# Attention rebuilt around transposed q and k: two heads per step on the two halves of the PE rows

## The chip, the cores and the metric

One core of one Trainium2 chip runs the whole program. The metric is device time in microseconds (us), the median of several executions. TensorE is PE in the profile (its weight loads are PEld), VectorE is DVE, ScalarE is ACT, GpSimd is POOL, and SyncE, which issues most of the DMAs, is SP.

## The reference

Three stages run after each other on B = 2 batches of S = 768 tokens. Only the first changes. It is attention with H = 8 heads of D = 64, n_global = 8 and n_local = 96:

```python
scores = scale * np.matmul(q, k.transpose(0, 1, 3, 2))
is_global = pos[None, :] < int(n_global)
is_local = (rel >= 0) & (rel < int(n_local))
keep = is_global | is_local
dist = np.where(is_global & ~is_local, float(n_local), np.abs(rel))
scores = np.where(keep, scores - slopes * dist, -1000000000.0)
a = np.exp(scores - np.max(scores, axis=-1, keepdims=True))
a = a / (np.sum(a, axis=-1, keepdims=True) + 1e-09)
return np.matmul(a, v)
```

The result x (1536 rows of 512) then goes through a mixer (x + x U V along the sequence, a layer of 512 to 2048 to 512) and through a layer of 8 experts of which each token takes one.

## The kernel before

**Attention** works on 8 pairs of heads. A pair has 6 blocks of 128 queries, and each block of each head is one step: STEPS = 12 steps a pair, 96 in all. A query block t > 0 looks at a window of 256 keys: the first 32 keys (which hold the global ones), the last 96 keys of block t - 1, and the 128 of block t. Block 0 has 128 keys. All engines run the same loops (`pairs`: two counted loops with two pairs in the body) and wait on semaphores whose values are computed in registers.

q and k arrive with tokens on the partitions. `load_qk` brings a pair in rows of 64 numbers, `turn_qk` transposes it on PE (L1156, 12 transposes a pair), and `keep_qk` copies it out of PSUM twice: ACT writes the fp32r rounding (L1244, L1247), and DVE writes the remainder (L1339, L1344). k is written once per window, so that each step finds its 256 keys side by side. q has a copy for each head in which the other head's 64 rows are zero, so that every score matmul contracts over 128 rows.

A step then runs so:

- `scores` on PE: three fp32r passes (high by high, high by low, low by high; `passes`, L452) of 128 x 256 into one of two PSUM banks.
- `score` on DVE (L1356): adds the bias of the head (from POOL, L1494) and takes the row minimum of the negated scores.
- `exponentials` on ACT (L1254), which also accumulates the row sums (the read of the accumulator is an instruction of its own).
- `turn_probs` on PE, TURN_LAG = 2 steps later: two fp32 transposes (L1173).
- `keep_turned`: a copy out of PSUM, on ACT for one head (L1261), on DVE for the other (L1364).
- `weigh` on PE, WEIGH_LAG = 4 steps later: two fp32 matmuls with 64 columns of v (L1189, L1190). The trace shows an fp32 matmul as two weight loads and two matmuls.
- twice a pair, `invert` and `normalise` (L1383) on DVE write the quotient to x.

Beside this POOL splits one unit of w_ch1 (128 x 1024) a pair into rounding (L1477) and remainder (L1479) and issues the DMA of the next unit itself.

**At the start** POOL builds index tiles, DVE turns n_global and n_local into numbers (L1306 to L1316; `path_ready`), then makes the distance tile in ten operations (L1319 to L1329; `dist_done`), and POOL multiplies it by each head's slope. With n_global up to 32 and n_local up to 97 the engines take the windowed path; it is the one that runs here.

**After attention** PE starts the mixer with 12 fp32 matmuls (L496), once `attn_done` is set. The mixer and the experts are not touched by the change, but for where the split units of w_ch1 come from.

Of the kernel before, what the change touches and what calls it, by code (L numbers as in the profile page):

```python
# [11 lines left out]
F32 = mybir.dt.float32  # L12
F32R = mybir.dt.float32r
# [30 lines left out]
def build(nc, q, k, v, n_global, n_local, moe_U, moe_V, w_ch1, w_ch2, w_gate, w_local, w1, w2, out):  # L44
    B, H, S, D = q.shape
# [4 lines left out]
    R = moe_U.shape[1]  # L50
# [13 lines left out]
    WIN = 2 * P  # L64
    HALF = TB // 2
    STEPS = 2 * TB
    CREDIT = STEPS + 1
    TURN_LAG = 2
    WEIGH_LAG = 4
    BATCHES = 4  # L70
# [6 lines left out]
    with ExitStack() as ctx:  # L77
# [17 lines left out]
        limits = sb("limits", [P, 2, 2], I32)  # L95
# [7 lines left out]
        qs = sb("qs", [P, TB, 2, D], F32, attn)  # L103
        ks = sb("ks", [P, TB, 2, D], F32, attn)
        vs = [sb(f"vs{i}", [P, TB, 2 * D], F32, attn) for i in range(2)]
        va = [sb(f"va{i}", [P, TB - 1, 2 * D], F32, attn) for i in range(2)]

        q_parts = sb("q_parts", [P, 2, 2, 2, S], F32R, attn)
        dist = sb("dist", [P, 3 * P], F32, attn)
        bias = [[sb(f"bias{i}{h}", [P, 3 * P], F32, attn) for h in range(2)] for i in range(2)]  # L110
        TS = [sb(f"TS{i}", [P, WIN], F32, attn) for i in range(3)]
        PR = [sb(f"PR{i}", [P, WIN], F32, attn) for i in range(3)]
        PT = [sb(f"PT{i}", [P, WIN], F32, attn) for i in range(4)]
        low = sb("low", [P, 2, STEPS], F32, attn)
        total = sb("total", [P, 2, STEPS], F32, attn)
        inv = sb("inv", [P, 2, STEPS], F32, attn)
        attn.close()
        (glob, near), (rel, key) = bias

        full = ExitStack()  # L120
        f_q = sb("f_q", [P, 2, D], F32, full)
        f_k = sb("f_k", [P, TB, 2, D], F32, full)
        f_v = sb("f_v", [P, TB, 2, D], F32, full)
# [20 lines left out]
        k_parts = sb("k_parts", [P, 2, 2, TB, WIN], F32R, turned_k)  # L144
# [63 lines left out]
        cleared = sem("cleared")  # L208
        setup = sem("setup")
        q_in = sem("q_in")  # L210
        k_in = sem("k_in")
        v_in = [sem(f"v_in{i}") for i in range(2)]
        bias_ready = sem("bias_ready")
        tr_done = sem("tr_done")
        tr_act = sem("tr_act")
        tr_dve = sem("tr_dve")
# [58 lines left out]
        raw_first = sem("raw_first")  # L275
# [5 lines left out]
        score_bank, turn_bank, out_bank, tr_bank = bank[0:2], bank[2:4], bank[4:6], bank[6:8]  # L281


        def width(s):
            return P if s < 2 else WIN

        def windows(dst, src, half, part):


            of = src.rearrange("p (t n) -> p t n", t=HALF)  # L290
            t0, t1 = HALF * half, min(HALF * (half + 1), TB - 1)
            if part == 0:
                yield dst[:, t0:t0 + HALF, P:WIN], of
                return
            yield dst[:, t0 + 1:t1 + 1, GLOB:P], of[:, 0:t1 - t0, P - SPAN:P]
            if half == 0:
                yield dst[:, 1:TB, 0:GLOB], of[:, 0:1, 0:GLOB].to_broadcast([P, TB - 1, GLOB])

        def pairs(eng, body):


            with eng.Fori(0, B) as b:
                with eng.Fori(0, H // 4) as g:
                    m = b * (H // 4) + g
                    for par in range(2):
                        body(b, g, m, par, 2 * m + par)

        LAST = B * H // 2 - 1
        PASSES = B * H // 4


# [14 lines left out]
        def full_sp(sp):  # L326
            def load(t, b, g, m):
                wait_loop(sp, f_free, m + 1)
                for h in range(2):
                    head = 2 * g + h  # L330
                    view = "a p t d -> p (a t) d"
                    for dst, src in ((f_k, k), (f_v, v)):
                        sp.dma_start(dst[:, :, h, :], src.rearrange("b h (t p) d -> (b h) p t d", p=P)[
                            bass.ds(b * H + head, 1), :, :, :].rearrange(view)).then_inc(f_in, 16)
                    sp.dma_start(f_q[:, h:h + 1, :], q.rearrange("b h (t p) d -> (b h t) p d", p=P)[
                        bass.ds((b * H + head) * TB + t, 1), :, :].rearrange("a p d -> p a d")).then_inc(f_in, 16)

            full_steps(sp, load)

        def full_pe(pe):  # L340
            def step(t, b, g, m):
                wait_loop(pe, f_in, 96 * (m + 1))
                pe.transpose(bank[0][:, 0:P], f_q[:, :, :].rearrange("p h d -> p (h d)"), ident[:, :])
                for i in range(TB):
                    last = pe.transpose(bank[1 + i // 4][:, (i % 4) * P:(i % 4 + 1) * P],
                                        f_k[:, i, :, :].rearrange("p h d -> p (h d)"), ident[:, :])
                last.then_inc(f_pe, 1)
                for h in range(2):
                    part = slice(h * D, (h + 1) * D)
                    if h == 0:  # L350
                        wait_loop(pe, f_dve, FULL_T * (t + 1) + FULL * m + 3)
                    else:
                        wait_loop(pe, f_dve, FULL_T * (t + 1) + FULL * m + 3 + FULL_H)
# [1178 lines left out]
```

## Time and profile before

| | |
|---|---|
| median of 3 runs | 689.23 us (688.92 to 689.52) |
| span of the profiled execution | 689.6 us |
| attention, from the first score matmul to x | 21.41 to 137.58 us |
| mixer from | 138.34 us |
| PE busy, weight loads busy | 90%, 79% of the span |

The span runs from the first to the last instruction of the profiled execution. Its rows are in microseconds from that start. The end of a matmul is modelled in such a profile; the starts are what to count with.

### The profile page before, as it was taken

Reading aid. Unit: us, or ns where it says so; the run is one execution under the profiler, and the core shown is the slowest. Engines: PE = TensorE matmul, PEld = TensorE weight load, DVE = VectorE, ACT = ScalarE, POOL = GpSimd, SP = SyncE. Lnnn points to the kernel's source line nnn. Section 1 sums busy time; section 2 is a strip of 40 time slices with the busy share of each in tenths; the row PEclk is TensorE's granted clock in tenths of the full one; section 3 lists DMA queues with packets and bytes.
Section 4 is the critical chain, followed back from the end, with each engine's and each line's share of the span. In section 5 each row is a group of like instructions: output and inputs, shape, how many; then the busy total and the mean of one; then the engine's idle time right before and its main releaser. Section 6 shows DMA issues by size and latency. Waiting matters only on the chain.

```text
span 689.6 us, 11540 instructions
## 1 busy us (share of the span) xinstructions
PE 621.2 (90%) x3430; PEld 541.6 (79%) x3431; DVE 308.2 (45%) x670; ACT 254.1 (37%) x554; POOL 96.6 (14%) x145
## 2 busy tenths in 40 slices
PE   0899899989999999999999999925899998999994
PEld 0789889938999998989998999824677876887883
DVE  5688888624332212220222011483665447574521
ACT  1677788613221111111111201321655346464411
POOL 6634433000000000000000000001112111212111
PEclk9999999999999999999999999955999999999998
DMA  8965676001111100010001000234684528654310
GB/s 209 201 151 118 135 150 142 1 0 62 61 62 62 47 0 1 1 46 1 1 1 46 1 1 1 72 126 151 209 284 155 185 70 284 242 200 159 115 43 21
DMA packets 72175, 65.78 MB, mean 95 GB/s; under 512 B 53807, under 2 KB 53807, under 8 KB 72144
## 3 DMA queue, kind: packets, MB, share of 16 engines
q1 hardware_dynamic: 64800, 50.87, 25.3%
q0 software_dynamic: 4320, 13.90, 6.3%
q10 hardware_dynamic: 3024, 0.61, 0.6%
q8 instruction: 18, 0.29, 0.2%
q14 instruction: 13, 0.11, 0.1%
HBM read 59.07 MB, written 7.08 MB: 96 GB/s over the span
## 4 chain that ended last, share of the span: by engine, by line
PE 82%; DVE 6%; issue 4%; DMA 3%; ACT 2%; SPq 1%; DVEq 0%; POOL 0%; ACTq 0%; POOLq 0%
PE bank L452 65%; PE bank L900 3%; PE bank L1173 2%; PE bank L1190 2%; PE bank L496 2%; PE bank L1156 2%; DMA raw<-in_moe_w_dram 2%; PE bank L1189 2%; ACT hs L955 1%; DVE q_parts L1339 1%; PE bank L515 1%; PE bank L524 1%; DVE wbuf L595 1%; PE bank L844 1%; DMA limits<-in_n_local_dram 1%
## 5 line engine op out<-in xcount | busy, mean ns | idle before, releaser
L452 PE MATMUL bank<-uT,wbuf 128*128 128x384 f32 x768 | 144.8, 336 | 1.5 <-DVE uT L670 1.5
L452 PE MATMUL bank<-wbuf,hid 128*128 128x512 f32 x576 | 145.1, 396 | 0.0
L452 PEld LDWEIGHTS bank<-uT,wbuf 128*128 128x128 f32 x768 | 136.2, 188 | 7.0 <-issue 1.7
L703 DVE SCALAR_TENSOR_TENSOR hid<-bank,hid 128x384 fp32r<-128x384 f32 x64 | 35.7, 557 | 214.9 <-ACT hid L644 214.9
L452 PEld LDWEIGHTS bank<-wbuf,hid 128*128 128x128 f32 x576 | 106.0, 188 | 20.6 <-issue 0.7
L644 ACT ACTIVATE hid<-bank 128x384 fp32r<-128x384 f32 x64 | 31.5, 492 | 230.0 <-PE bank L452 230.0
L595 DVE TENSOR_TENSOR wbuf<-raw,wbuf 128x1024 fp32r<-128x1024 f32 x72 | 85.1, 1221 | 27.3 <-ACT wbuf L591 26.5
L452 PE MATMUL bank<-wbuf,xT 128*128 128x512 f32 x360 | 93.1, 410 | 1.7 <-DVE xT L985 1.7
L591 ACT CAST wbuf<-raw 128x1024 fp32r<-128x1024 f32 x72 | 72.9, 1047 | 41.4 <-PE bank L452 20.4
L452 PE MATMUL bank<-wbuf,hT 128*128 128x512 f32 x360 | 86.0, 394 | 0.0
L452 PEld LDWEIGHTS bank<-wbuf,xT 128*128 128x128 f32 x360 | 69.6, 197 | 16.3 <-issue 2.1
L452 PEld LDWEIGHTS bank<-wbuf,hT 128*128 128x128 f32 x360 | 66.6, 189 | 13.5
L452 PE MATMUL bank<-k_parts,q_parts 128*128 128x256 f32 (+1 forms) x288 | 57.9, 312 | 2.0 <-DVE k_parts L1344 2.0
L1254 ACT ACTIVATE PR<-TS,low 128x256 f32<-128x256 f32 (+1 forms) x96 | 47.3, 492 | 25.9 <-DVE low L1356 24.1
L1356 DVE CUSTOM_DVE_ANT_0 TS<-bank,bias 128x256 f32<-128x256 f32 (+1 forms) x96 | 38.1, 397 | 19.3 <-PE bank L452 13.4
L1020 POOL IOTA rev<- 128x96 f32 x1 | 0.3, 288 | 323.6 <-PE bank L452 323.6
L452 PEld LDWEIGHTS bank<-k_parts,q_parts 128*128 128x128 f32 x288 | 41.6, 196 | 2.5 <-issue 2.4
L1173 PE MATMUL bank<-ident,PR 128*128 128x128 f32 x176 | 36.5, 281 | 0.2
L955 ACT ACTIVATE hs<-bank 128x512 f32<-128x512 f32 x30 | 17.9, 597 | 46.1 <-PE bank L452 44.5
L1055 POOL DMA_INDIRECT out_dram<-ys,give x15 | 16.1, 1075 | 108.3 <-DVE ys L1011 108.3
L1190 PE MATMUL bank<-vs,PT 128*128 128x64 f32 x160 | 30.9, 275 | 0.0
L997 DVE TENSOR_TENSOR hT<-bank,hT 128x512 fp32r<-128x512 f32 x30 | 20.7, 689 | 21.6 <-ACT hT L961 21.4
(177 smaller groups left out, 622.1 us busy)
## 6 DMA issues: line engine op xcount, KB each, us to landing
raw<-in_moe_w_dram SPq DMA_DIRECT2D x64, 512.0 KB, 4.1
raw<-in_moe_w_ch_dram POOLq DMA_DIRECT2D x12, 512.0 KB, 5.9
qs<-in_q_dram SPq DMA_DIRECT2D x16, 192.0 KB, 5.5
ks<-in_k_dram SPq DMA_DIRECT2D x16, 192.0 KB, 4.5
vs<-in_v_dram SPq DMA_DIRECT2D x16, 192.0 KB, 2.6
mixed<-x SPq DMA_DIRECT2D x12, 256.0 KB, 2.1
raw<-in_moe_w_ch_dram SPq DMA_DIRECT2D x4, 512.0 KB, 3.5
va<-in_v_dram SPq DMA_DIRECT2D x16, 120.0 KB, 4.1
```

The costliest lines, as they stand in the source:

```text
L452: last = pe.matmul(dst, lhs[a], rhs[b_], start=start and i == 0, stop=stop and i == 2)
L591: act.copy(w[:, 0, i, :], raw[:, i % RAW, :]).then_inc(hi_split, 1)
L595: dve.tensor_tensor(w[:, 1, i, :], raw[:, i % RAW, :], w[:, 0, i, :].bitcast(F32), ALU.subtract).then_inc(lo_split, 1)
L644: act.activation(hid[i % 2][:, 0, :], bank[3 + i % 2][:, 0:BN], ACT.Relu).then_inc(hid_hi, 1)
L703: dve.scalar_tensor_tensor(hid[i % 2][:, 1, :], bank[3 + i % 2][:, 0:BN], 0.0, hid[i % 2][:, 0, :].bitcast(F32), ALU.max, ALU.subtract).th ...
L900: last = pe.transpose(bank[5 + half][:, c * P:(c + 1) * P], hs[:, half, c * P:(c + 1) * P], ident[:, :])
L955: act.activation(hs[:, half, :], bank[3 + half][:, :], ACT.Relu).then_inc(e_relu, 1)
L997: dve.tensor_tensor(hT[:, 1, half * NE // 2:(half + 1) * NE // 2, :], bank[5 + half][:, :].rearrange("p (c t) -> p c t", c=NE // 2), hT[:, ...
L1173: last = pe.transpose(turn_bank[s % 2][:, c * P:(c + 1) * P], PR[s % 3][:, c * P:(c + 1) * P], ident[:, :])
L1190: last = pe.matmul(dst, PT[s % 4][:, P:WIN], vs[par][:, t, vcol], start=False, stop=True)
L1254: act.activation(PR[s % 3][:, 0:w], TS[s % 3][:, 0:w], ACT.Exp, bias=low[:, par, s:s + 1], scale=-1.0, accum_out=total[:, par, s:s + 1]).t ...
L1356: dve.tensor_tensor_reduce(TS[s % 3][:, 0:w], score_bank[s % 2][:, 0:w], bias[par][s % 2][:, col], -SCALE, 3.0e38, ALU.add, ALU.min, low[: ...
```

## The change

The host hands over other layouts: q and k of a pair transposed (128 rows: head 0 on partitions 0 to 63, head 1 on 64 to 127), v with a column of ones behind each head and with the shifted windows already laid out, both limits and both gates in one array each. On the chip:

- Both heads of a query block are one group: 6 groups a pair, 48 in all, written out without loops; waits are on constants.
- `turn_qk` and `keep_qk` are gone. POOL makes rounding and remainder of q and k from SBUF (`split_qk`); for the first 256 columns of the first pair ACT and DVE do it.
- A score matmul contracts over the 64 rows of its head. The keys are not copied into windows: for t > 0 each pass is a matmul of 32 keys and one of 224, for each head, so a group has 12 score matmuls (6 at t = 0) into two PSUM banks, of four.
- The row sums come from the ones column of v in the `weigh` matmuls (65 columns), so `exponentials` no longer accumulates, and the reciprocal is part of `normalise`.
- `keep_turned` copies both heads at once (512 columns), on ACT for four groups of six, on DVE for two.
- The roundings of w_ch1 are made by ACT (`first_hi`); POOL makes only the remainders, and SP issues their DMAs.
- The distance tile takes five DVE operations, of which four come behind the limits.

```diff
+            def load_qk(n):
+                sp.dma_start(k_raw[n % 2][:, :], kT[n, :, :]).then_inc(qk_in[n % 2], 16)
+                sp.dma_start(q_raw[n % 2][:, :], qT[n, :, :]).then_inc(qk_in[n % 2], 16)
+
+            def load_v(n):
+                sp.dma_start(vs[n % 2][:, :], vw[n, :, :]).then_inc(v_in[n % 2], 16)
+
+            def load_first(i):
+
+                sp.wait_ge(pool_split, i + 1)
+                load_raw(sp, i + RAW)
+
+            load_qk(0)
+            load_v(0)
+            load_qk(1)
+            for u in range(RAW):
+                load_raw(sp, u)
+            sp.dma_start(u_sb[:, :, :, :], moe_U).then_inc(const_in, 16)
+            sp.dma_start(v_raw[:, :], moe_V).then_inc(const_in, 16)
...
+            def scores(g):
+                n, t = divmod(g, TB)
+                par = n % 2
+                if t == 0:
+                    if n == 0:
+                        pe.wait_ge(lo_first, 2)
+                    else:
+                        pe.wait_ge(parts, 4 * (n + 1))
+                if g == 2:
+                    pe.wait_ge(parts, 4)
+                late_enough(pe, scored, 2 * g - 2)
+                spans = ((0, slice(0, P)),) if t == 0 else ((0, slice(0, GLOB)), (GLOB, slice((t - 1) * P + GLOB, (t + 1) * P)))
+                first = True
+                for a, b_ in ((0, 0), (0, 1), (1, 0)):
+                    for at, keys in spans:
+                        for h in range(2):
+                            part = slice(h * D, (h + 1) * D)
+                            dst = score_bank[2 * (g % 2) + h][:, at:at + keys.stop - keys.start]
+                            last = pe.matmul(dst, q_parts[part, par, a, t * P:(t + 1) * P], k_parts[part, par, b_, keys],
+                                             start=first, stop=a == 1, skip_group_check=True)
+                        first = False
+                last.then_inc(qk_done, 1)
...
+            def weigh(g):
+                n, t = divmod(g, TB)
+                par, half = n % 2, t // HALF
+                pe.wait_ge(*((pt_dve, dve_copies(g)) if copied_by_dve(t) else (pt_act, act_copies(g))))
...
+                    pe.wait_ge(v_in[par], 16 * (n // 2 + 1))
+                if t % HALF == 0:
+                    late_enough(pe, normed, 2 * (n - 1) + half + 1)
+                for h in range(2):
+                    at = (t % HALF) * VW + h * (D + 1)
+                    dst = out_bank[half][:, at:at + D + 1]
+
+                    def values(i):
+                        return vs[par][:, i * VW + h * (D + 1):i * VW + (h + 1) * (D + 1)]
+
+                    if t == 0:
+                        last = pe.matmul(dst, PT[g % 3][:, h, 0:P], values(0), start=True, stop=True)
+                    else:
+                        pe.matmul(dst, PT[g % 3][:, h, 0:P], values(TB + t - 1), start=True, stop=False)
+                        last = pe.matmul(dst, PT[g % 3][:, h, P:WIN], values(t), start=False, stop=True)
                 last.then_inc(pv_done, 1)
...
+                for g in range(GROUPS + WEIGH_LAG):
+                    if g < GROUPS:
+                        scores(g)
+                    if 0 <= g - TURN_LAG < GROUPS:
+                        turn_probs(g - TURN_LAG)
+                    if g >= WEIGH_LAG:
+                        weigh(g - WEIGH_LAG)
...
+            def exponentials(g):
+                w = width(g % TB)
+                late_enough(act, turned, g - 2)
+                for h in range(2):
+                    act.wait_ge(scored, 2 * g + h + 1)
+                    act.activation(PR[g % 3][:, h, 0:w], TS[g % 3][:, h, 0:w], ACT.Exp, bias=low[:, g, h:h + 1],
+                                   scale=-1.0).then_inc(exped, 1)
+
+            def keep_turned(g):
+                t = g % TB
+                if copied_by_dve(t):
+                    return
+                w = width(t)
+                act.wait_ge(turned, g + 1)
+                late_enough(act, pv_done, g - 2)
+                act.copy(PT[g % 3][:, :, 0:w], turn_bank[g % 2][:, :].rearrange("p (h n) -> p h n", h=2)[:, :, 0:w]
+                         ).then_inc(pt_act, 1)
+
+            def first_hi(i):
+                raw_ready(act, i)
+                act.copy(wbuf[0][:, 0, i, :], raw[:, i % RAW, :]).then_inc(first_split, 1)
...
+            dve.wait_ge(dist_ready, 5)
+            link(dve.tensor_scalar(far, rel, 0.0, None, ALU.is_lt))
...
+
+            dve.wait_ge(qk_in[0], 32)
+            link(dve.tensor_copy(q_parts[:, 0, 0, 0:WIN], q_raw[0][:, 0:WIN]))
+            dve.tensor_tensor(q_parts[:, 0, 1, 0:WIN], q_raw[0][:, 0:WIN], q_parts[:, 0, 0, 0:WIN].bitcast(F32),
+                              ALU.subtract).then_inc(lo_first, 1)
+            dve.wait_ge(hi_first, 2)
+            dve.tensor_tensor(k_parts[:, 0, 1, 0:WIN], k_raw[0][:, 0:WIN], k_parts[:, 0, 0, 0:WIN].bitcast(F32),
+                              ALU.subtract).then_inc(lo_first, 1)
+
+            out_of_reach = -MASKED * 2.0 ** 8
+            link(dve.tensor_scalar(key, key, ng, out_of_reach, ALU.is_ge, ALU.mult))
+            link(dve.scalar_tensor_tensor(reach, rel, nl, far, ALU.is_ge, ALU.max))
+            link(dve.scalar_tensor_tensor(reach, reach, out_of_reach, rel, ALU.mult, ALU.add))
+            dve.scalar_tensor_tensor(dist[:, :], key, nl, reach, ALU.max, ALU.min).then_inc(dist_done, 1)
+
+            def score(g):
+                n, t = divmod(g, TB)
+                w = width(t)
+                col = slice(0, P) if t == 0 else slice(P, 3 * P)
+                dve.wait_ge(qk_done, g + 1)
+                late_enough(dve, exped, 2 * (g - 2))
+                for h in range(2):
+                    head = 2 * n + h
+                    if t == 0 and head < H:
+                        dve.wait_ge(bias_ready, head + 1)
+                    dve.tensor_tensor_reduce(TS[g % 3][:, h, 0:w], score_bank[2 * (g % 2) + h][:, 0:w],
+                                             bias[:, head % H, col], -SCALE, 3.0e38, ALU.add, ALU.min,
+                                             low[:, g, h:h + 1]).then_inc(scored, 1)
+
+            def keep_turned(g):
+                t = g % TB
+                if not copied_by_dve(t):
+                    return
+                dve.wait_ge(turned, g + 1)
+                late_enough(dve, pv_done, g - 2)
+                dve.tensor_copy(PT[g % 3][:, :, :].rearrange("p h n -> p (h n)"), turn_bank[g % 2][:, :]).then_inc(pt_dve, 1)
+
+            def normalise(n, half):
+                b, u = divmod(n, PAIRS // B)
+                at = 2 * (2 * n + half)
+                of = out_bank[half][:, 0:HALF * VW].rearrange("p (t h d) -> p t h d", h=2, d=D + 1)
+                each = inv[:, :].rearrange("p (t h o) -> p t h o", h=2, o=1)
+                dve.wait_ge(pv_done, TB * n + HALF * (half + 1))
+                dve.tensor_scalar(each, of[:, :, :, D:D + 1], 1.0e-9, None, ALU.add).then_inc(inv_step, 1)
+                dve.wait_ge(inv_step, at + 1)
+                dve.reciprocal(inv[:, :], inv[:, :]).then_inc(inv_step, 1)
+                dve.wait_ge(inv_step, at + 2)
+                dst = x[:, b * TB + half * HALF:b * TB + (half + 1) * HALF, u * 2 * D:(u + 1) * 2 * D]
+                dve.tensor_tensor(dst.rearrange("p t (h d) -> p t h d", h=2), of[:, :, :, 0:D],
+                                  each.to_broadcast([P, HALF, 2, D]), ALU.mult).then_inc(normed, 1)
 
...
+            def split_qk(n):
+                par = n % 2
+                cols_n = slice(WIN if n == 0 else 0, S)
+                pool.wait_ge(qk_in[par], 32 * (n // 2 + 1))
+                late_enough(pool, qk_done, TB * (n - 1))
+                for of, to in ((q_raw, q_parts), (k_raw, k_parts)):
+                    pool.tensor_copy(to[:, par, 0, cols_n], of[par][:, cols_n]).then_inc(parts, 1)
+                pool.wait_ge(parts, 4 * n + 2)
+                for of, to in ((q_raw, q_parts), (k_raw, k_parts)):
+                    pool.tensor_tensor(to[:, par, 1, cols_n], of[par][:, cols_n], to[:, par, 0, cols_n].bitcast(F32),
+                                       ALU.subtract).then_inc(parts, 1)
+
+            def split_first(i):
+                pool.wait_ge(first_split, i + 1)
+                pool.tensor_tensor(wbuf[0][:, 1, i, :], raw[:, i % RAW, :], wbuf[0][:, 0, i, :].bitcast(F32),
+                                   ALU.subtract).then_inc(pool_split, 1)
+
+            def prepare_bias(h):
+                pool.tensor_tensor(bias[:, h, :], dist[:, :], slopes[:, h:h + 1].to_broadcast([P, 3 * P]),
+                                   ALU.mult).then_inc(bias_ready, 1)
+
...
-                pairs(pool, prepare)
+                for n in range(PAIRS):
+                    if 2 * n < H:
+                        prepare_bias(2 * n)
+                        prepare_bias(2 * n + 1)
+                    if n + 1 < PAIRS:
+                        split_qk(n + 1)
+                    split_first(n)
             with pool.Else():
                 full_pool(pool, split_first)
...
+    def turned(a):
+        return a.transpose(0, 1, 3, 2).reshape(pairs, 2 * d, s)
+
+    own = v.reshape(pairs, 2, tb, P, d).transpose(0, 3, 2, 1, 4)
+    windows = _np.concatenate([_np.repeat(own[:, :GLOB, 0:1], tb - 1, 2), own[:, GLOB:, :tb - 1]], 1)
+    padded = _np.ones((pairs, P, 2 * tb - 1, 2, d + 1), v.dtype)
+    padded[..., :d] = _np.concatenate([own, windows], 2)
```

## Rows read from the trace of the kernel before

**Rows 1.** The page: its span, and busy us of each engine.

```profile
span 689.6 us, 11540 instructions
...
PE 621.2 (90%) x3430; PEld 541.6 (79%) x3431; DVE 308.2 (45%) x670; ACT 254.1 (37%) x554; POOL 96.6 (14%) x145
```

**Rows 2.** Busy time by stretch: length, busy (x instructions) of PE PEld DVE ACT POOL, clock.

```profile
42.90:57.36 14.46, 13.37 (x115) 12.89 (x115) 12.48 (x46) 11.38 (x40) 5.56 (x5) 1.00 0.61 144
...
122.43:136.73 14.30, 14.11 (x123) 13.68 (x122) 9.55 (x43) 9.45 (x35) 0.00 (x0) 1.00 0.00 0
21.30:26.30 5.00, 4.50 (x20) 4.32 (x21) 1.25 (x7) 1.99 (x8) 3.41 (x4) 1.00 1.29 230
```

**Rows 3.** Timeline of the weight loads (PEld) of one step: start us, us, instruction.

```profile
63.37 0.42 PEld L452 LDWEIGHTS bank<-k_parts,q_parts 128*128 128x128 f32 x3
...
63.74 0.24 PEld L1173 LDWEIGHTS bank<-ident,PR 128*128 128x128 f32 x2
...
63.95 0.30 PEld L1189 LDWEIGHTS bank<-va,PT 128*128 128x128 f32 x2
...
64.17 0.30 PEld L1190 LDWEIGHTS bank<-vs,PT 128*128 128x128 f32 x2
...
64.40 0.41 PEld L452 LDWEIGHTS bank<-k_parts,q_parts 128*128 128x128 f32 x3
...
64.42 0.53 PE L452 MATMUL bank<-k_parts,q_parts 128*128 128x128 f32 x3
```

**Rows 4.** Timeline of PE: a turn of k, in brackets the idle time before it.

```profile
57.34 0.55 PE L1156 MATMUL bank<-ident,ks 128*128 128x128 f32 x3 [0.97 <-DVE q_parts L1339]
```

**Rows 5.** Groups by form, 0 to 175 us, TensorE: count, busy us, mean ns.

```profile
L452 PE MATMUL bank<-k_parts,q_parts 128*128 128x256 f32 x240 | 48.8, 313 | 0.0
L452 PEld LDWEIGHTS bank<-k_parts,q_parts 128*128 128x128 f32 x288 | 41.6, 196 | 2.5 <-issue 2.4
...
L1173 PEld LDWEIGHTS bank<-ident,PR 128*128 128x128 f32 x176 | 20.5, 141 | 1.8 <-ACT PT L1261 0.3 <-issue 0.2 <-ACT PR L1254 0.2
```

**Rows 6.** The chain that ended last, at the end of attention: start us, us.

```profile
137.01 0.57 DVE x L1383
...
138.34 12.25 PE bank L496 x24
```

**Rows 7.** Timeline from the start to the first scores.

```profile
6.20 2.54 DVE L1306 CAST lim<-limits 128x2 f32<-128x2 int32 x1 [6.06 <-DMA limits<-in_n_local_dram]
...
10.15 0.15 DVE L1316 CAST flags<-lim 128x1 int32<-128x1 f32 x1
...
15.17 0.56 DVE L1329 TENSOR_TENSOR dist<-dist,bias 128x384 f32<-128x384 f32 x1
...
17.30 1.61 POOL L1494 TENSOR_TENSOR bias<-dist,slopes 128x384 f32<-128x384 f32 x2 [5.57 <-issue]
...
21.41 1.61 PE L452 MATMUL bank<-k_parts,q_parts 128*128 128x128 f32 x6 [1.97 <-DVE k_parts L1344]
...
23.31 0.29 DVE L1356 CUSTOM_DVE_ANT_0 TS<-bank,bias 128x128 f32<-128x128 f32 x1 [0.38 <-PE bank L452]
```

**Rows 8.** The page's DMA issues: KB each, median us from issue to landing.

```profile
raw<-in_moe_w_dram SPq DMA_DIRECT2D x64, 512.0 KB, 4.1
```

**Rows 9.** Groups by form, 0 to 175 us, the other engines.

```profile
L1254 ACT ACTIVATE PR<-TS,low 128x256 f32<-128x256 f32 x80 | 40.8, 510 | 17.5 <-DVE low L1356 16.8
...
L1356 DVE CUSTOM_DVE_ANT_0 TS<-bank,bias 128x256 f32<-128x256 f32 x80 | 33.5, 418 | 13.1 <-PE bank L452 11.0 <-ACT PR L1254 1.0
...
L1479 POOL TENSOR_TENSOR wbuf<-raw,wbuf x8 | 19.0, 2374 | 2.2 <-POOL wbuf L1477 2.2
...
L1477 POOL CAST wbuf<-raw x8 | 8.3, 1034 | 2.7 <-DMA raw<-in_moe_w_ch_dram 2.7
...
L670 DVE TENSOR_TENSOR uT<-bank,uT 128x512 fp32r<-128x512 f32 x3 | 1.9, 683 | 0.2 <-ACT uT L621 0.2
...
L621 ACT CAST uT<-bank 128x512 fp32r<-128x512 f32 x3 | 1.8, 586 | 2.8 <-PE bank L515 2.8
```

More of the change, by code:

```diff
@@ L278, in build, with width, copied_by_dve, act_copies @@
         y_out = sem("y_out")
[L281 to L309, printed above, removed]
+        score_bank, turn_bank, out_bank = bank[0:4], bank[4:6], bank[6:8]
+        def width(t):
+            return P if t == 0 else WIN
+        def copied_by_dve(t):
+            return t % HALF == HALF - 1
+        def act_copies(g):
+            return sum(not copied_by_dve(i % TB) for i in range(g + 1))
+        def dve_copies(g):
+            return g + 1 - act_copies(g)
+        def late_enough(eng, sem_, value):
+            if value > 0:
+                eng.wait_ge(sem_, value)
         def path(eng):
@@ L1223, in _ @@
         def _(act):
-            for i in range(3):
-                act.dma_start(u_sb[:, :, i, :], moe_U.rearrange("(t p) r -> p t r", p=P)).then_inc(const_in, 16)
-                act.dma_start(v_raw[i * R:(i + 1) * R, :], moe_V).then_inc(const_in, 16)
-            with nc.allow_non_contiguous_dma(reason="the gates' few columns"):
-                act.dma_start(gate_sb[:, :, 0:E], w_gate.rearrange("(c p) e -> p c e", p=P)).then_inc(const_in, 16)
-            act.sem_inc(exped, 3)
-            act.sem_inc(pt_act, 1)
@@ L1429, in _ @@
+            with dve.If(path(dve)):
+                for g in range(GROUPS + HALF + 2):
+                    if g < GROUPS:
+                        score(g)
+                    if 0 <= g - TURN_LAG < GROUPS:
+                        keep_turned(g - TURN_LAG)
+                    if g >= TB and g % HALF == 0 and g - WEIGH_LAG < GROUPS:
+                        normalise(*divmod((g - TB) // HALF, 2))
+                normalise(PAIRS - 1, 1)
+                dve.wait_ge(normed, 2 * PAIRS)
             with dve.Else():
@@ L1461, in _ @@
             last.then_inc(dist_ready, 1)
-            for par in range(2):
-                pool.memset(q_parts[:, par, :, :, :].bitcast(F32), 0.0).then_inc(cleared, 1)
-            for i in range(RAW):
-                c, j = divmod(i, FF // UNIT)
-                pool.dma_start(raw[:, i, :], w_ch1[c * P:(c + 1) * P, j * UNIT:(j + 1) * UNIT]).then_inc(raw_first, 16)
-            with nc.allow_non_contiguous_dma(reason="the local gate's one column"):
-                pool.dma_start(gate_sb[:, :, E:NG], w_local.rearrange("(c p) e -> p c e", p=P)).then_inc(y_out, 16)
```

509 lines of the change are left out of this document (153 added, 356 removed).

## The prediction

> **What bounds the kernel now.** I read the page first. PE is busy for 621.2 of 689.6 us, and no other engine for half of the span [rows 1]: the end is set by what PE does and by what it waits for. The change touches attention only. The chain of waits shows its end: the last quotient is written at 137.0 to 137.6 us, and PE starts the mixer at 138.3 [rows 6]. What stands behind that, 552 us, stays as it is, so the question is when attention ends.
>
> Second, the stretches: a pair of heads takes 14.46 us, in which PE records 115 matmuls and as many weight loads, while DVE is busy 12.5, ACT 11.4 and POOL 5.6 us. The last pair, with no transposes of q and k beside it, issues 122 loads in 14.3 us [rows 2]. Third, the timeline of one step, to see what PE's time is made of. Its nine loads run from 63.37 to 64.40: 1.03 us, 0.114 us for each. It doesn't matter that the score matmuls have 256 columns and those of v have 64 [rows 3]. So **attention costs PE a weight load of 0.114 us per matmul**, and columns below 256 are free. The code has 114 loads a pair, 912 in all (288 of them for scores, 176 for transposed probabilities [rows 5], 352 for v, 96 to transpose q and k). 912 x 0.114 is 104 us of the 115.6 us from 21.4 to 137.0 [rows 6, 7]. The other 11.6 are the start, where 20 matmuls need 5 us [rows 2] and not 2.3, and waits in front of the transposes of k, such as 0.97 us behind DVE's last write of q_parts [rows 4]. The clock row says 1.00 for these first 5 us, but each load takes twice as long as later; I keep that cost in both kernels.
>
> **The change, part by part.**
>
> *Start.* Before, both heads' first scores are through DVE at 23.7 us [rows 7], after: limits, ten distance operations, transposes and copies of q and k. Now: the limits land as before, at about 5 to 6 us. DVE's first operation of the kernel took 2.54 us [rows 7], and now falls into the wait for them. Its small operations take 0.195 us each (eight from 8.74 to 10.30 [rows 7]), so seven of them end at 7. q and k of a pair are 393 KB each in rows of 3 KB; 512 KB units land 4.1 us after their issue [rows 8], so both are there by about 6.5. Three splits of 256 columns (0.4 each, as half of 512 columns at 0.68 [rows 9]) end at 8.2, four distance operations (ten took the 5.4 us from 10.3 to 15.7 [rows 7]; I take 0.62 each) at 10.7. Before, POOL's bias started 1.57 us behind `dist_done`, and two took 1.61 [rows 7]; so with the path's branch ahead of them the two biases end at 13.1 and 13.9, and the first group is through DVE at 14.3. POOL's own split of 512 columns of q and k (two casts at half of 1.03, two subtractions at half of 2.37: 3.4 us [rows 9]) ends at 10, under that cover. **Gain 9.4 us**; between 7 and 11, as the landing times are estimates.
>
> *Weight loads.* Transposes of q and k go: 96 loads fewer. Transposed probabilities and v stay at 176 and 352 (65 columns are as free as 64). Scores go from 3 loads a step to 6 a head and group: 5 x 12 + 6 = 66 a pair, 528 in all instead of 288. One by one the sum is 1056. But head 0's loads and matmuls use rows 0 to 63 of the array, and head 1's the other half. If those of a pair overlap, the scores cost as much as 264 loads, and the sum is 792. The trace has no matmul on half of the rows, so both ends stand: **792 or 1056 loads, 90.3 or 120.4 us against 104**. A matmul of 128 columns is as fast as one of 256 in these rows (three in 0.53 us, against a spacing of 0.114 a load [rows 3]), so I take 32 and 224 columns to be hidden behind their loads too.
>
> Which end? In these rows the next load already runs while the last matmul does (a load lasts 0.19 us and starts every 0.114 [rows 3, 5]), so PE overlaps what doesn't collide, and two halves of the array don't. I take the overlap at 65 in 100. The Trainium skill ("TensorE: Matmul & The Clock Gate", Part 3: Packing small matmuls) says that matmuls in distinct row groups start within 4 ns of each other, and gives 3.07 times the speed for four groups of 32 rows with 512 columns; no run here shows it yet, and with 512 columns a load is hidden anyway.
>
> *The seams between halves and whole.* Each group goes from whole-array matmuls to halves and back: 96 seams, which the kernel before hasn't. Lower bound nothing. Upper bound: the next load waits until the last matmul is out of the array. A matmul is recorded at 0.28 us (0.313 for 256 columns [rows 5]), and normally the next starts 0.11 after it, so 0.17 us a seam, 16 us in all. I take the middle, **8 us**. The Trainium skill ("TensorEngine Tiling (Array Packing)", Key Properties) speaks against the change here: a change of tiling mode drains the engine. By that rule the sum would be 8 us above mine, and by overlap without a drain 8 below.
>
> *The other engines, for each pair.* ACT: twelve exponentials of at most 0.51, four copies of at most 0.59, one cast of a 1024 wide unit, estimated at twice a 512 wide one's 0.59 less its fixed part, 1.1: 9.6 us at most. DVE: twelve scores of 0.42 with 0.08 behind each, my estimate, 6.0, two copies of 0.68, two normalisations of some 0.95 (the quotient of 384 columns and two small operations): 9.3. POOL: two biases 1.6, two casts of 768 columns 1.6, two subtractions 3.6, one of 1024 columns 2.4: 9.1 for the first four pairs [rows 7, 9]. All lie under PE's 99 x 0.114 + 1 = 12.3. Lags are a whole group longer than each chain: probabilities are wanted two groups (4 us) after their scores, and the way through DVE and ACT takes 2.2. What queues up is POOL: the bias of the next pair stands behind its subtraction for w_ch1, and this behind a cast that ACT makes after its fourth group. That is ready some 13 us into the pair, as DVE asks for it at 12.5: 0 to 1 us for three pairs, taken as 0 because PE has a group of slack.
>
> *DMA.* v comes with 5.7 KB a row, q and k with 3 KB, where rows of 256 bytes stood. Nothing waited for data in the middle before, so this is worth nothing but the start. SP now waits for POOL's remainder ahead of the loads of the next v; each has 10 us to come.
>
> **The sum.** First group through DVE at 14.3; 792 - 9 = 783 loads of 0.114 are 89.3; the slow first 5 us cost 2.7; the first probabilities come 1 us late; the seams 8; the last quotient as before 0.9 behind the last matmul. That is 116.2 instead of 137.6: 21.4 us less. The rows are of an execution with a span of 689.6 us, the median is 689.2, so the forecast is **668 us**.
>
> **The rivals.**
> 1. *Overlap and free seams*: 116.2 - 8 = 108.2, time 660 us. For it: in the rows of one step no load starts late. Chance 0.2. With full drains 676; half-way 668. My case reaches from 662 to 676, chance 0.42.
> 2. *Halves run one after another, seams free*: the loads are 1056 - 18 = 1038, 118.3 us instead of 89.3, time 660 + 29 = 689 us: no change. The gain at the start pays for more loads. For it: loads are what limits PE here, and each may use one path into the array, whichever rows it fills. Chance 0.1.
> 3. *One after another, and each seam drains*: 689 + 8 to 689 + 16, time 697 to 705 us: slower. This decides as soon as both heads' loads don't overlap and a seam costs over 0.01 us. Chance 0.17.
> 4. *Another engine sets the pace*: one wait per group for DVE or ACT of 0.2 us, or POOL's late bias. Then a pair takes 13.3 us rather than 12.3, and the time is 668 + 8 = 676 to 684 us. Against it: 9 to 10 us of work in 12. Chance 0.11.
>
> **The numbers.** Faster by over 0.2% (which is about what a measurement can tell from none): my case, the first and the fourth, 0.73, and a bit of the second where seams and start come out well, 0.03: 0.76. Within 0.2%: 0.04. Slower: the third and the rest of the second, 0.20. The range reaches from 655 (the first with 2 us less at the start and fewer waits) to 692 (the second, with its start 3 us worse); it leaves out the drains of the third.
>
> **What would show it.** In the profile after: the first DVE score of both heads by 14 to 15 us. In the timeline of a group, starts of the score loads of head 0 and head 1: pairs within a few ns mean overlap, 0.11 apart means none. Behind the last score matmul of a group, a gap of 0.17 us before the next load would be a drain. A pair of 12.3 us, and the mixer's first matmul at 117 us with the 551 us after it unchanged. The prediction is wrong if a pair takes over 14 us, or if matmuls of 32 and 224 columns need more than their loads.

## The result: 749.5 us, 8.8% slower, with attention at TensorE's lower clock from end to end

The changed kernel takes 749.52 us (median of 4 executions, 746.93 to 751.23) beside 689.38 us for the one before; the ratio is 1.088, with a 95% interval of 1.084 to 1.092. I had forecast 668.

The page and the end of attention in the chain of waits, after the change, beside [rows 1, 6]:

```profile
span 748.4 us, 10131 instructions
...
PE 694.2 (93%) x3574; PEld 605.7 (81%) x3575; DVE 267.9 (36%) x562; ACT 225.7 (30%) x380; POOL 109.7 (15%) x147
```

```profile
197.77 0.57 DVE x L1322
...
199.12 3.96 PE bank L488 x5
```

The mixer starts at 199.1 us instead of 138.3: all of the loss is in attention, 60.8 us. Behind it stand 748.4 - 199.1 = 549.3 us, as good as the 689.6 - 138.3 = 551.3 before. Now the start, as a timeline, beside [rows 7]:

```profile
4.33 0.17 DVE L1264 CAST lim<-limits 128x4 f32<-128x4 int32 x1 [1.03 <-DMA limits<-in_limits_dram]
...
6.31 1.26 POOL L1375 TENSOR_TENSOR q_parts<-q_raw,q_parts 128x512 fp32r<-128x512 f32 x1
6.47 1.38 DVE L1277 TENSOR_TENSOR q_parts<-q_raw,q_parts 128x256 fp32r<-128x256 f32 x1
7.53 1.44 POOL L1375 TENSOR_TENSOR k_parts<-k_raw,k_parts 128x512 fp32r<-128x512 f32 x1
7.77 1.48 DVE L1280 TENSOR_TENSOR k_parts<-k_raw,k_parts 128x256 fp32r<-128x256 f32 x1
...
10.86 0.62 DVE L1287 SCALAR_TENSOR_TENSOR dist<-TS,lim 128x384 f32<-128x384 f32 x1
12.47 1.61 POOL L1384 TENSOR_TENSOR bias<-dist,slopes 128x384 f32<-128x384 f32 x2 [2.77 <-DVE dist L1287]
...
14.11 0.29 DVE L1299 CUSTOM_DVE_ANT_0 TS<-bank,bias 128x128 f32<-128x128 f32 x1 [0.36 <-POOL bias L1384]
```

The first group is through DVE at 14.4 us, where I had put 14.3. So the loss comes after 14.4 us. The weight loads of one group, as a timeline of PEld, beside [rows 3]:

```profile
80.52 0.55 PEld L1184 LDWEIGHTS bank<-vs,PT 128*128 128x128 f32 x2
80.94 0.55 PEld L1185 LDWEIGHTS bank<-vs,PT 128*128 128x128 f32 x2
81.37 0.55 PEld L1184 LDWEIGHTS bank<-vs,PT 128*128 128x128 f32 x2
81.80 0.55 PEld L1185 LDWEIGHTS bank<-vs,PT 128*128 128x128 f32 x2
82.46 1.35 PEld L1150 LDWEIGHTS bank<-k_parts,q_parts 64*128 64x128 f32 x12
84.01 0.29 PEld L1163 LDWEIGHTS bank<-ident,PR 128*128 128x128 f32 x2 [0.20 <-issue]
```

Two loads for v take 0.43 us, so one comes every 0.213 us, where it was 0.11 before: twice as long, for instructions that the change hasn't touched. That is the lower of the clock's two levels, 1.2 GHz and not 2.4. The 12 loads of the scores end 1.35 us after the first starts; 12 in a row at 0.213 would take 2.6. So the two heads' loads do run side by side. From one full group to the next it takes 4.19 us (score loads at 66.40 and 70.59 us in the same timeline). The counts by stretch, beside [rows 2]:

```profile
20.00:40.00 20.00, 20.00 (x115) 18.43 (x114) 5.83 (x25) 7.30 (x17) 9.10 (x7) 1.00 0.09 30
...
140.00:160.00 20.00, 20.00 (x117) 18.40 (x118) 5.96 (x27) 6.22 (x15) 5.20 (x5) 1.00 0.20 64
```

114 and 118 loads in 20 us at the start and near the end: the stream is slow from the first group to the last, and no other engine is near its limit. The clock column prints 1.00 here, as it did for the slow first 5 us of [rows 2], since the trace has no entry of the clock before its first rise. That rise is behind attention, at some 202 us, during the 512-column matmuls of the mixer. Where a rise came earlier in the same execution, the column is right (run e7 below: 0.50, with 113 loads in 20 us).

### The profile page after: what moved, and what is told of

It reads as the page before. It is cut to its first block, busy times and chain, and to the rows that moved or that the text cites. A ratio compares the mean times of both kernels' runs of the same rounds, so it can differ in the third digit from the quotient of the medians.

```text
span 748.4 us, 10131 instructions
## 1 busy us (share of the span) xinstructions
PE 694.2 (93%) x3574; PEld 605.7 (81%) x3575; DVE 267.9 (36%) x562; ACT 225.7 (30%) x380; POOL 109.7 (15%) x147
## 3 DMA queue, kind: packets, MB, share of 16 engines
q1 hardware_dynamic: 22080, 57.83, 22.4%
## 4 chain that ended last, share of the span: by engine, by line
PE 89%; DVE 4%; DMA 2%; ACT 2%; issue 2%; POOL 0%; POOLq 0%; DVEq 0%; ACTq 0%; SPq 0%
PE bank L444 56%; PE bank L1150 9%; PE bank L1163 6%; PE bank L1185 5%; PE bank L1184 4%; PE bank L889 2%; PE bank L488 2%; DMA raw<-in_w_dram 1%; ACT hs L944 1%; PE bank L507 1%; PE bank L516 1%; PE bank L1182 1%; DVE wbuf L587 1%; PE bank L833 1%; DMA xs<-mixed,take 1%
## 5 line engine op out<-in xcount | busy, mean ns | idle before, releaser
L1150 PE MATMUL bank<-k_parts,q_parts 64*128 64x32 f32 (+2 forms) x528 | 71.8, 416 | 12.3 <-DVE k_parts L1280 9.3
L1299 DVE CUSTOM_DVE_ANT_0 TS<-bank,bias 128x256 f32<-128x256 f32 (+1 forms) x96 | 34.8, 400 | 115.4 <-PE bank L1150 113.1
L1150 PEld LDWEIGHTS bank<-k_parts,q_parts 64*128 64x128 f32 x528 | 59.8, 322 | 17.7 <-DVE k_parts L1280 9.0
L1216 ACT ACTIVATE PR<-TS,low 128x256 f32<-128x256 f32 (+1 forms) x96 | 41.9, 485 | 30.3 <-DVE low L1299 30.3
L1185 PE MATMUL bank<-vs,PT 128*128 128x65 f32 x160 | 50.5, 417 | 0.0
L1163 PE MATMUL bank<-ident,PR 128*128 128x128 f32 x176 | 49.9, 432 | 0.0
L1184 PE MATMUL bank<-vs,PT 128*128 128x65 f32 x160 | 46.3, 392 | 0.0
L1226 ACT COPY PT<-bank 128x512 f32<-128x512 f32 (+1 forms) x32 | 17.0, 532 | 93.3 <-PE bank L1163 93.3
L1185 PEld LDWEIGHTS bank<-vs,PT 128*128 128x128 f32 x160 | 43.7, 333 | 0.0
## 6 DMA issues: line engine op xcount, KB each, us to landing
v_raw<-in_V_dram SPq DMA_DIRECT2D x1, 288.0 KB, 12.9
```

What stands on the lines that cost most here:

```text
L1150: last = pe.matmul(dst, q_parts[part, par, a, t * P:(t + 1) * P], k_parts[part, par, b_, keys], start=first, stop=a == 1, skip_group_check ...
L1163: last = pe.transpose(turn_bank[g % 2][:, at:at + P], PR[g % 3][:, h, c * P:(c + 1) * P], ident[:, :])
L1184: pe.matmul(dst, PT[g % 3][:, h, 0:P], values(TB + t - 1), start=True, stop=False)
L1185: last = pe.matmul(dst, PT[g % 3][:, h, P:WIN], values(t), start=False, stop=True)
L1216: act.activation(PR[g % 3][:, h, 0:w], TS[g % 3][:, h, 0:w], ACT.Exp, bias=low[:, g, h:h + 1], scale=-1.0).then_inc(exped, 1)
L1226: act.copy(PT[g % 3][:, :, 0:w], turn_bank[g % 2][:, :].rearrange("p (h n) -> p h n", h=2)[:, :, 0:w]).then_inc(pt_act, 1)
```

## The experiments

Theory H (history): the clock is low because nothing ahead of this stream raised it, and would stay high once raised. Theory A (activity): the stream couldn't hold the high clock either. Beside that: which part of the change takes away what raised the clock before. Only e12 was timed in several executions (6); each other run is one execution. The kernel before lay between 684.5 and 692.6 us in 11 executions timed beside e12, so single runs tell differences of ten us and more, and not of two or three.

**e1_warm: a burst ahead of attention.** In the changed kernel:

```diff
+            def heat(count):
+                for _ in range(count):
+                    pe.matmul(bank[7][:, :].rearrange("p (a n) -> p a n", a=4), ones[:, :],
+                              ones[:, :].rearrange("p (a n) -> p a n", a=1).to_broadcast([P, 4, P]), start=True, stop=True)
+
+            heat(4)
...
                 for g in range(GROUPS + WEIGH_LAG):
+                    if g == 2:
+                        heat(4)
```

> The kernel after the change, with 4 fp32 matmuls of 512 columns on PE before attention and 4 more behind the scores of the second group, while PE would wait for the bias. Their results are overwritten. Theory H (history): the low clock of the attention stage is kept only because PE never was busy enough ahead of it, and once raised it holds. Then loads come every 0.11 us, a pair takes some 12.5 us and the time is 665 to 680 us. Theory A (activity): attention's own stream of matmuls is too thin in this form, whatever came before; the clock falls back soon after the burst and the time is 745 to 757 us.

664.1 us: 85 us less from eight added matmuls. H holds, A falls; e12 repeats it.

**e2_whole_rows, e3_before_half_rows, e4_before_narrow: parts alone, without a burst.** e2 is the changed kernel with `part = slice(0, P)` in `scores`. e3 is the kernel before with q and k cut to the rows of the step's head. e4 is the kernel before with 32 and 224 columns:

```diff
-                passes(pe, dst[:, 0:width(s)], [q_parts[:, par, a, h, t * P:(t + 1) * P] for a in range(2)],
-                       [k_parts[:, par, a, t, WIN - width(s):WIN] for a in range(2)], True, True).then_inc(qk_done, 1)
+                spans = ((0, P),) if s < 2 else ((0, GLOB), (GLOB, WIN))
+                first = True
+                for a, b_ in ((0, 0), (0, 1), (1, 0)):
+                    for lo, hi in spans:
+                        last = pe.matmul(dst[:, lo:hi], q_parts[:, par, a, h, t * P:(t + 1) * P],
+                                         k_parts[:, par, b_, t, WIN - width(s) + lo:WIN - width(s) + hi],
+                                         start=first, stop=a == 1, skip_group_check=True)
+                        first = False
+                last.then_inc(qk_done, 1)
```

> The kernel after the change, with every score matmul over all 128 rows instead of the 64 of its head (so both heads get the sum of both heads' scores: the output differs). As many matmuls with the same columns, but nothing overlaps and no change between halves and whole. Theory R (rows or seams: half-array matmuls, or the holes at the seams, keep the clock low): the clock is granted within the first pairs, loads every 0.11 us, 1056 of them: 690 to 700 us. Theory C (columns: the many matmuls of 32 columns keep it low): loads every 0.213 us one by one, 8 x 132 x 0.213 = 225 us of attention, about 790 us.

> The kernel before, with one part of the change alone: each score matmul contracts over the 64 rows of its head. Nothing overlaps, since the three passes of a step belong to one head; each step has two seams. Theory R: the clock isn't granted in attention, 912 loads of 0.213 us and seams: 790 to 810 us. Theory C: the clock is granted as before, and only 192 seams of 0.07 to 0.12 us are added: 700 to 715 us.

> The kernel before, with another part of the change alone: each score pass of 256 columns in two matmuls, of 32 and 224 columns, over all 128 rows. 240 loads more. Theory C: the clock isn't granted in attention, 1152 loads of 0.213 us, 810 to 830 us. Theory R: the clock is granted, 240 loads of 0.11 us more: 713 to 718 us.

786.5, 804.3 and 812.9 us: none of the three raises the clock in attention. Their stretches from 60 to 80 us, e2, e3 and e4:

```profile
60.00:80.00 20.00, 20.00 (x97) 20.00 (x96) 5.18 (x23) 5.72 (x13) 3.50 (x3) 1.00 0.21 77
60.00:80.00 20.00, 20.00 (x83) 16.99 (x82) 9.03 (x32) 7.90 (x27) 4.79 (x4) 1.00 0.21 47
60.00:80.00 20.00, 20.00 (x98) 20.00 (x98) 8.80 (x32) 8.29 (x29) 2.18 (x3) 1.00 0.26 59
```

96 and 98 loads over all rows in 20 us are one every 0.2 us, which is the lower level; e3's 82 have the seams of every step between them. Each edit of e3 and e4 alone was enough to lose the high clock, so neither R (rows or seams) nor C (columns) alone is the answer. The kernel before can't have stood far from losing it itself.

**e5_contiguous: pairs and seams as changed, but wide matmuls.**

```diff
-                spans = ((0, slice(0, P)),) if t == 0 else ((0, slice(0, GLOB)), (GLOB, slice((t - 1) * P + GLOB, (t + 1) * P)))
+                spans = ((0, slice(0, P)),) if t == 0 else ((0, slice((t - 1) * P, (t + 1) * P)),)
```

> The kernel after the change, without a burst, but with each score pass in one matmul of 256 adjacent keys (block t - 1 and block t) in place of 32 and 224: the first 32 keys of the sequence are not looked at, so the output differs. Pairs of heads and seams stay. If the narrow matmuls are what keeps the clock from rising, it rises within the first groups, 99 - 15 = 84 loads a pair in time: 645 to 655 us. If halves and seams are enough to keep it low: 84 loads of 0.213 us and seams a pair, 17.5 to 20.5 us, 715 to 730 us.

655.1 us, with no burst. In the chain of waits four transposes of probabilities take 1.04 us and then 0.59, and 367 loads fit into 40 us later on:

```profile
17.22 1.04 PE bank L1163 x4
19.34 0.59 PE bank L1163 x4
```

```profile
60.00:100.00 40.00, 40.00 (x369) 35.73 (x367) 25.88 (x116) 27.89 (x62) 22.49 (x15) 1.00 0.40 136
```

The clock rises 4 us into the stream, at 18.4 us, and holds. Paired halves with their seams don't keep it down here. But two things went at once, the narrow matmuls and their loads (84 load times a pair, not 99); e11, e14 and e15 take them apart.

**e7_warm_ahead_only and e8_warm_behind_only: one half of the burst.**

> The kernel after, with the first burst only (4 matmuls, which end at about 9.8 us; PE then has 1.2 us of scores and waits until 14.3). The clock is raised in the burst. Does it hold over the wait? If it holds: 663 to 667 us. If it falls there and attention can't raise it: 745 to 752 us.

> The kernel after, with the second burst only: 4 matmuls from about 11 us, at the low clock 1.7 us each, so to 17 or 18, some 3 us past the point at which the scores could go on. If 6 us of dense matmuls raise the clock: 666 to 670 us. If they don't: 750 to 756 us.

746.1 and 667.5 us. Stretches of e7, then its PE timeline:

```profile
4.00:9.00 5.00, 5.00 (x8) 1.73 (x6) 4.32 (x10) 0.41 (x1) 3.69 (x4) 1.00 1.01 393
20.00:40.00 20.00, 20.00 (x114) 18.48 (x113) 5.82 (x25) 7.48 (x17) 9.11 (x7) 0.50 0.09 30
```

```profile
9.48 1.27 PE L1157 MATMUL bank<-k_parts,q_parts 64*128 64x128 f32 x18 [0.27 <-DVE k_parts L1287]
14.73 1.62 PE L1157 MATMUL bank<-k_parts,q_parts 64*128 64x32 f32 x12 [3.98 <-DVE low L1306]
```

The burst raised the clock; PE then stood 4 us behind the second group's scores, waiting for the bias, and when it went on the clock was down (0.50). It stayed so until 191.9 us, when only the last transposes and matmuls with v were left. The first group after the pause already takes 1.62 us for its scores. So a raised clock is of use only if it lasts into attention: behind this pause of 4 us it was gone, while e8's burst ran into the scores without one.

**e6_before_warm: is the burst a gain by itself?** Bursts of 8, 4 and 2 ahead of, between and behind the first transposes of the kernel before.

> The kernel before, with bursts of 8, 4 and 2 fp32 matmuls of 512 columns on PE ahead of, between and behind the first transposes of q and k, where PE waits. If a high clock from the first score on is all that the burst gives, the slow first 5 us become 2.3: 685 to 689 us, and the burst in the changed kernel isn't worth its 85 us by itself but only together with the change. If the burst helps in other ways (the clock drop behind attention too), 680 to 686 us.

689.0 us beside 688.4: no difference that these runs can tell. The kernel before raises its clock without help, so the burst is worth something only where the stream doesn't. Even here the clock fell once more, at 24.4 us, just behind a pause of 1.16 us in which PE waited for q, and the stream of 256-column scores had it up again at 27.8 us.

**e9_before_narrow_warm and e10_before_half_warm: e4 and e3 with those bursts.**

> e4_before_narrow with the bursts of e6_before_warm (8, 4 and 2 matmuls ahead of the first scores). If a raised clock holds for this stream too: 240 loads of 0.11 us more than before, 27 us: 713 to 718 us. If narrow score matmuls can't even hold it: 800 us and more.

> e3_before_half_rows with the same bursts. Held: seams at the high clock alone, 192 of 0.09 and 0.17 us, 25 us, less what steps had to wait anyway: 700 to 715 us. Not held: 795 us and more. This is the price of unpaired halves, where the changed kernel's are paired.

788.4 and 701.2 us. Their stretches from 60 to 80 us, e9 and then e10:

```profile
60.00:80.00 20.00, 20.00 (x98) 20.00 (x98) 8.55 (x31) 7.82 (x26) 2.59 (x3) 0.50 0.24 55
```

```profile
60.00:80.00 20.00, 20.00 (x144) 16.66 (x143) 15.55 (x57) 15.17 (x51) 5.69 (x5) 1.00 0.59 146
```

e10 holds the high clock with a stream that, started low in e3, never reached it. (The clock fell here too, at 19.0 us, and the last burst had it up again at 22.4, as the scores began.) That is H again, in the other kernel. Unpaired halves cost it 701.2 - 689.0 = 12 us, from one execution of each. In e9 the clock fell at 24.9 us, 1.2 us behind a pause of 1.47 us in which PE waited for q:

```profile
23.74 0.54 PE L1163 MATMUL bank<-ident,qs 128*128 128x128 f32 x3 [1.47 <-DMA qs<-in_q_dram]
```

The bursts are those of e6, and the pause and the fall come within 0.5 us of where they come there. In e6 256-column scores had the clock up again some 3 us later; here, with 32 and 224 columns, it took until 212.6 us. That pair is the plainest evidence that the split of the score passes is what holds the rise back. But the clock did come back, in the middle of the same stream and with nothing new on PE, and then held to the end of attention:

```profile
190.00:212.00 22.00, 22.00 (x108) 22.00 (x108) 8.80 (x34) 8.50 (x27) 5.69 (x5) 0.50 0.21 57
213.00:233.00 20.00, 20.00 (x184) 20.00 (x182) 12.28 (x52) 12.45 (x44) 0.00 (x0) 1.00 0.00 0
```

108 loads in 22 us, then 182 in 20: that is why e9 takes 24 us less than e4 and less than the 800 I expected. So the narrow stream raises the clock rarely rather than never; it didn't in the 240 us of e4, and why it did here no run shows. Whether the pause or the narrow matmuls lost the clock at 24.9 us e9 doesn't tell by itself; e6 lost it there with wide ones, and from 213 us on, as in e13, narrow matmuls over whole rows hold it.

**e11_wider: 256 and 32 columns instead of 224 and 32**, the three wide passes first.

> The kernel after, without a burst: for t > 0 the three passes over 256 adjacent keys come first, then three of 32 keys write over the first 32 columns. The scores are the same, the matmuls and loads as many, but 288 columns stream in place of 256 a pass and head. If the columns for each load alone decide, this lies between the kernel after (128 on average, low) and e5_contiguous (256, raised), and may go either way: 660 us if it rises within the first 10 us, 750 to 765 us if it doesn't. If the order matters (three wide ones in a row), it rises.

744.4 us, with 116 loads from 60 to 80 us: the clock stays low. As many matmuls and loads as in the changed kernel and 32 columns more a pass, with the wide ones in a row, aren't enough.

**e12_warm_timed: the kernel of e1 in more executions.**

> The kernel of e1_warm again, timed against the one before. If the clock comes up with the burst in every execution: 663 to 666 us each time, a ratio of 0.963. If it depends on luck, some executions lie at 745 us.

667.7 us, median of 6 (666.5 to 669.6); the ratio to the kernel before is 0.969, interval 0.965 to 0.972. With all six within 3.1 us, the clock comes up in every execution. In the profiled one the clock falls for a moment behind attention, as in the kernel before; in e1's it doesn't, which is the 1.7 us between them in the mixer's first 24 matmuls (12.25 us here, 10.55 in e1). Loads of one group, a stretch, and the end of attention in the chain:

```profile
60.71 0.42 PEld L1170 LDWEIGHTS bank<-ident,PR 128*128 128x128 f32 x4
61.09 0.30 PEld L1191 LDWEIGHTS bank<-vs,PT 128*128 128x128 f32 x2
61.31 0.30 PEld L1192 LDWEIGHTS bank<-vs,PT 128*128 128x128 f32 x2
61.54 0.30 PEld L1191 LDWEIGHTS bank<-vs,PT 128*128 128x128 f32 x2
61.76 0.30 PEld L1192 LDWEIGHTS bank<-vs,PT 128*128 128x128 f32 x2
62.13 0.74 PEld L1157 LDWEIGHTS bank<-k_parts,q_parts 64*128 64x128 f32 x12
62.99 0.42 PEld L1170 LDWEIGHTS bank<-ident,PR 128*128 128x128 f32 x4
```

```profile
60.00:80.00 20.00, 20.00 (x211) 18.28 (x210) 10.75 (x48) 11.93 (x28) 12.89 (x10) 1.00 0.38 131
```

```profile
115.07 0.57 DVE x L1331
...
116.42 3.72 PE bank L488 x5
```

A load every 0.111 us, a group in 2.28 us (60.71 to 62.99), 210 loads in 20 us instead of 118, and the mixer at 116.4 us.

**e13_whole_rows_warm, e14_224_only, e15_wide_values.** e13 is e2 with the burst of e1. e14 leaves out the 32-column matmuls from the fourth group on. e15 leaves the scores alone and widens the matmuls with v:

```diff
-                    at = (t % HALF) * VW + h * (D + 1)
-                    dst = out_bank[half][:, at:at + D + 1]
+                    at = (t % HALF) * VW
+                    dst = out_bank[half][:, at:at + VW]
...
-                        return vs[par][:, i * VW + h * (D + 1):i * VW + (h + 1) * (D + 1)]
+                        return vs[par][:, i * VW:(i + 1) * VW]
```

> e2_whole_rows (score matmuls over all 128 rows, unpaired, no seams; the output differs) with the bursts of e1_warm. If the clock holds: 264 loads of 0.111 us more, 29 us, less 12 us of seams: 680 to 685 us, so that pairing and seams together are worth 13 to 20 us. If it doesn't hold: about 785 us.

> The kernel after, without a burst, and from the fourth group on without the 32-column matmuls (the first 32 keys are not looked at, stale scores stand in their place; the output differs). Half as many score matmuls, 224 columns for each. If the many short loads with 32 columns keep the clock low, it rises here as in e5_contiguous: 652 to 660 us. If not: 715 to 725 us.

> The kernel after, without a burst, scores unchanged, but each matmul with v takes both heads' 130 columns instead of its 65 and writes them to the same place (head 1's write over head 0's; the output differs). Its two passes of 130 columns stream for about as long as a weight load takes, so it costs almost nothing. If columns per load over the whole stream decide: the clock rises in the first 10 us, 665 to 672 us. If it is the score matmuls themselves that are too narrow: 745 to 755 us.

683.6, 723.7 and 693.9 us. In e14 the clock stays low with 224 columns for each score load, so the 32-column matmuls aren't the cause as such. From the fourth group on e14 has the matmuls and loads of e5 but for 32 of 256 columns a pass, so the loads that e5 saved aren't what raised its clock. As the first three groups differ too, and each ran once, this pair shows how near the edge is and not where it lies. Two stretches of e15:

```profile
20.00:30.00 10.00, 10.00 (x60) 9.03 (x59) 2.97 (x15) 3.49 (x7) 8.12 (x7) 1.00 0.25 83
40.00:50.00 10.00, 10.00 (x106) 8.98 (x102) 5.10 (x25) 4.81 (x12) 8.34 (x7) 1.00 0.32 109
```

59 loads in 10 us, then 102: the clock rises at about 30 us and holds, later than I expected, and the added columns are in another kind of matmul, with as many loads as in the changed kernel. So the scores as such aren't what the clock hangs on: what they lack can be given back elsewhere in the stream. In e13, at the high clock, a stretch of 40 us:

```profile
60.00:100.00 40.00, 40.00 (x364) 40.00 (x362) 20.32 (x91) 22.53 (x49) 20.27 (x14) 1.00 0.45 154
```

362 loads of 0.11 us one after another. Whole rows with narrow matmuls do hold the clock here. The time is 683.6 beside 667.7 and 664.1 of e12 and e1: pairing, with its seams paid, is worth 16 us (beside e12, whose clock falls behind attention as e13's does) to 20.

## Why the prediction was wrong, step by step

- *Start.* The number is right, 14.4 us against 14.3, and in part by luck, since its terms were off both ways. DVE's small operations were over at 6.2 us instead of 7. Its two subtractions of 256 columns took 1.38 and 1.48 us where I had 0.4 each, while POOL's subtractions ran. POOL's bias then began 1.0 us behind the distance tile (11.48 to 12.47), where I had 1.6.
- *Loads and pairs.* Right: 792 load times. The 12 score loads of both heads take the time of 6, at either clock.
- *Seams.* Right in kind, 5 us too small: at the high clock a group takes 2.28 us for 18 load times of 0.1115, so two seams cost 0.27 us and all of them 13 us. I had 8, from a range of 0 to 16.
- *Other engines, DMA.* Right: at the high clock PE has almost no idle time between 15 and 115 us, and no other engine has more than POOL's 12.9 of 20 us from 60 to 80 us (ACT 11.9, DVE 10.8).
- *The sum* gives the mixer's start at 117 us. With the clock raised it is 116.4, and the time 664 to 668. That it fits so well is in part luck: the seams cost 5 us more, but the slow first 5 us (2.7) aren't there behind a burst, and a load took 0.1115 us instead of 0.114 (2 us). **What failed is the term "783 loads of 0.114 us"**, and behind it one clause: the slow first 5 us, "I keep that cost in both kernels". Each load took 0.213 us, a group 4.19 us, and the slow phase lasted 184 us instead of 5. I had seen that loads take twice as long at first, and never asked what ends that phase, and whether the change leaves that in place.
- *The rivals.* None of the four was this. The third forecast a slower kernel too, by 8 to 16 us, but from loads one after another, and they overlap. Its other condition held: the two seams of a group cost 0.27 us, 13 us in all.

What ended the slow phase before was the stream itself: whole-row matmuls of 256 columns. The change halves the score columns for each load, and e4 shows that this alone was enough to keep the clock low, and e9 beside e6 that it can delay a rise from 3 us to 188; e3 shows the same as e4 for halving the rows without pairing; e5 and e15 show that columns put back, in the scores or elsewhere, raise it. The Trainium skill ("TensorE: Matmul & The Clock Gate", Part 1: The HAM clock gate) says that the throttled state is the default and activity releases it; e1, e7 and e12 agree. What stays open is what exactly counts as activity: these runs order the streams, they don't measure the quantity, and but for the changed kernel itself (4 executions) and e12 (6) each is one execution. Nor did I try a raised clock for longer stages than this one.

## What to carry to other kernels

Weight loads that set PE's pace hide the columns that you save, but here the clock didn't come up without them: check of every thinner stream that it still brings the clock up, by counting loads in a stretch and not by the clock column ahead of its first entry. A stream that doesn't raise the clock may still hold it, so a few 512-column matmuls in a wait that is there anyway can be worth 80 us, if they run into the stream; behind a pause of 4 us (e7) the raised clock was gone. And if a slow phase at the start of a trace looks like a constant, find out what ends it before it goes into a sum for another kernel.

## What the runs showed of the hardware that I hadn't expected

- The same stream of attention ran for 184 us at the low clock after a cold start, and for 100 us at the high one after a burst; e8's 4.9 us of 512-column matmuls (11.56 to 16.39 us) were enough. The two levels are 82 us apart with the same instructions in attention.
- Fp32r matmuls on 64 rows each, for different heads and PSUM banks, load and run side by side: 12 score loads take the time of 6, 1.35 us at the low clock and 0.74 at the high one, against 2.6 and 1.3 one by one.
- Going from halves to whole rows and back costs 0.27 us a group at the high clock and 4.19 - 18 x 0.213 = 0.36 us at the low one.
- Subtractions with both operands in SBUF, on DVE and on POOL at the same time: DVE took 1.38 and 1.48 us for 256 columns, while 72 such operations of 1024 columns took 1.22 us on average behind attention. Each of the two ended 0.28 us behind POOL's (7.85 and 9.25 us against 7.57 and 8.97). The Trainium skill ("SBUF — State Buffer", SBUF: two separate sides) says that such an operation and one of GpSimd take an exclusive lock on a shared port pair; the times here agree with DVE having waited for POOL's.
